# A spectral filter and two expert layers: the last super-tile 498 columns wide, the first loads and products reordered, the last unit ordered for its stores

## The reference

```python
X = np.fft.rfft(x, axis=1)
y = np.fft.irfft(X * (filt_r + 1j * filt_i)[None], n=3008, axis=1)
t = y.reshape(6016, 256)                       # 6016 tokens
h = t @ w_in                                   # layer 1
t = np.where(h > 0, h, np.exp(np.minimum(h, 0)) - 1) @ w_out
h = t @ w2_in                                  # layer 2
out = (h * np.clip(h + 3, 0, 6) / 6) @ w2_out
```

## Time and profile before

| | |
|---|---|
| median of 3 runs | 1104.79 us (1104.62 to 1105.99) |
| the profiled execution's own time | 1103.63 us |
| its span in the trace | 1101.8 us |
| PE busy, DVE, ACT, POOL | 99%, 69%, 70%, 25% |

### The profile page before, as it was taken

The page is one execution under the profiler, slowest core; times in us unless marked ns, Lnnn a source line. Parts: engine busy times, 40 slices in busy tenths (PEclk is TensorE's granted clock), DMA queues, the critical chain, the costliest instruction groups (busy, mean ns, idle before and its releaser), DMA issues.

```text
span 1101.8 us, 13377 instructions
## 1 busy us (share of the span) xinstructions
PE 1093.9 (99%) x4798; PEld 882.8 (80%) x4798; DVE 757.3 (69%) x941; ACT 765.9 (70%) x1149; POOL 280.4 (25%) x215
## 2 busy tenths in 40 slices
PE   9999999999999999999999999999999999999998
PEld 4666878888888888888887888888888888888886
DVE  7998676666666676676687866665665666666665
ACT  0554788788788788888898666566666666666654
POOL 4757051111111111120398620120121021020000
PEclk9999999999999999999999999999999999999999
DMA  9755200200100101101211201001101001000001
GB/s 288 241 173 175 91 1 3 74 1 14 63 1 31 44 1 38 39 1 38 76 58 57 76 1 38 38 1 38 38 1 38 38 1 38 38 1 1 38 1 38
DMA packets 29330, 54.20 MB, mean 49 GB/s; under 512 B 3408, under 2 KB 19664, under 8 KB 29264
## 3 DMA queue, kind: packets, MB, share of 16 engines
q1 hardware_dynamic: 23648, 44.12, 12.0%
q10 hardware_dynamic: 5616, 9.22, 2.5%
HBM read 34.83 MB, written 18.51 MB: 48 GB/s over the span
## 4 chain that ended last, share of the span: by engine, by line
PE 91%; ACT 4%; DVE 2%; issue 1%; POOL 1%; ACTq 0%; POOLq 0%
PE ps L479 43%; PE ps L470 13%; PE ps L468 13%; PE ps L469 13%; PE ps L432 3%; PE ps L400 3%; PE ps L408 2%; DVE e L776 2%; PE ps L417 1%; ACT e L634 1%; ACT w_hi L606 1%; ACT e L636 1%; PE ps L419 1%; PE ps L420 1%; PE ps L438 0%
## 5 line engine op out<-in xcount | busy, mean ns | idle before, releaser
L790 DVE TENSOR_TENSOR g_lo<-e,g_hi 128x502 fp32r<-128x502 f32 (+1 forms) x288 | 276.5, 988 | 135.0 <-ACT g_hi L669 134.3
L468 PE MATMUL ps<-op_hi,w_hi 128*128 128x502 f32 x672 | 261.9, 390 | 0.0
L470 PE MATMUL ps<-op_lo,w_hi 128*128 128x502 f32 x672 | 261.8, 390 | 0.0
L469 PE MATMUL ps<-op_hi,w_lo 128*128 128x502 f32 x672 | 261.2, 389 | 0.0
L479 PE MATMUL ps<-g_lo,w_hi 128*128 128x502 f32 x766 | 236.9, 390 | 1.2 <-DVE g_lo L790 0.9
L479 PE MATMUL ps<-g_hi,w_hi 128*128 128x502 f32 x766 | 235.7, 389 | 0.2 <-ACT g_hi L669 0.2
L479 PE MATMUL ps<-g_hi,w_lo 128*128 128x502 f32 x766 | 234.9, 388 | 0.0
L873 POOL TENSOR_TENSOR op_lo<-op_raw,op_hi 128x1004 fp32r<-128x1004 f32 (+1 forms) x48 | 100.8, 2102 | 448.3 <-ACT op_hi L614 448.1
L479 PEld LDWEIGHTS ps<-g_lo,w_hi 128*128 128x128 f32 x766 | 143.3, 188 | 32.4 <-DVE g_lo L790 3.9
L479 PEld LDWEIGHTS ps<-g_hi,w_hi 128*128 128x128 f32 x766 | 143.7, 188 | 29.9 <-ACT g_hi L669 1.2
L479 PEld LDWEIGHTS ps<-g_hi,w_lo 128*128 128x128 f32 x766 | 144.1, 188 | 29.3
(11 more groups left out here) (74 smaller groups left out, 1147.9 us busy)
## 6 DMA issues: line engine op xcount, KB each, us to landing
op_raw<-y SPq DMA_DIRECT2D x36, 251.0 KB, 3.6
x_ring<-x_dev SPq DMA_DIRECT2D x32, 192.0 KB, 4.9
y<-ystage SPq DMA_DIRECT2D x12, 502.0 KB, 2.9
out_dev<-ystage SPq DMA_DIRECT2D x11, 502.0 KB, 2.9
y<-ystage ACTq DMA_DIRECT2D x18, 235.0 KB, 2.5
f_ring<-f_dev SPq DMA_DIRECT2D x11, 384.0 KB, 6.6
w_raw<-w_dev ACTq DMA_DIRECT2D x16, 256.0 KB, 4.5
w_raw<-w_dev SPq DMA_DIRECT2D x16, 256.0 KB, 3.1
```

Of the source, the lines that this page charges most:

```text
L468: pe.matmul(out, w_hi[p][:, cols], hi, start=start, stop=False, skip_group_check=True)
L469: pe.matmul(out, w_lo[p][:, cols], hi, start=False, stop=False, skip_group_check=True)
L470: pe.matmul(out, w_hi[p][:, cols], lo, start=False, stop=True, skip_group_check=True).then_inc(done, 1)
L790: return dve.tensor_tensor(g_lo[:, tiles, :], e[:, tiles, :], f32(g_hi[:, tiles, :]), ALU.subtract)
```

## The change

Four things change. (1) The last super-tile of each layer has two tiles of `LAST_T` = 498 columns; the padding, its memset and its store go, and the rows of `y0`, `y1` and the output are 6016 long. TensorE's matmuls, GpSimd's sums and the operand splits of that super-tile are 498 wide, ScalarE's and VectorE's work on the activations stays 502 wide. (2) The first `x` tile is loaded from ScalarE's queue ahead of the sign vector, the second takes its place on SyncE's, and the third zero product is 256 columns wide. (3) At `u` = 0 one of the two bank-filling products and the first `up` stand ahead of the wait for group 30. (4) The last unit runs 11, 21, and then 22 and 12 together, first for one output half, then for the other; the last half is stored in two transfers, partitions 0 to 63 from SyncE and 64 to 127 from ScalarE.

```diff
 T = 502
-TOKP = NS * 2 * T
-PAD = TOKP - TOK
+LAST_T = (TOK - (NS - 1) * 2 * T) // 2
...
+        def width(s):
+            return LAST_T if s % NS == NS - 1 else T
...
             sp.dma_start(mat("A"), mats_dev[:, 0:P]).then_inc(mat_loaded["A"], 16)
-            load_x(0)
+            load_x(1)
             sp.dma_start(mat("BX"), mats_dev[:, P:2 * P]).then_inc(mat_loaded["BX"], 16)
-            load_x(1)
             load_x(2)
...
-            sp.wait_ge(zeroed, 2)
-            sp.dma_start(y0[:, :, TOK:].rearrange("o p t -> p o t"), pad_zero[:]).then_inc(pad_stored, 16)
...
-            for o in range(DH):
-                sp.wait_ge(end_evac[o], 1)
-                sp.dma_start(out_dev[o, :, at:at + T], ystage[:, 1, o * T:o * T + T]).then_inc(y_stored[1], 16)
+            sp.wait_ge(end_evac[0], 1)
+            sp.dma_start(out_dev[0, :, at:at + LAST_T], ystage[:, 1, 0:LAST_T]).then_inc(y_stored[1], 16)
+            sp.wait_ge(end_evac[1], 1)
+            sp.dma_start(out_dev[1, 0:P // 2, at:at + LAST_T],
+                         ystage[0:P // 2, 1, T:T + LAST_T]).then_inc(y_stored[1], 16)
...
-            for _ in range(3):
-                pe.matmul(ps[:, 0, :], back[:, 0, 0, :], back[:, 0, 0:4, :].rearrange("p j d -> p (j d)"),
-                          start=True, stop=True)
+            for cols in (4, 4, 2):
+                pe.matmul(ps[:, 0, 0:cols * P], back[:, 0, 0, :],
+                          back[:, 0, 0:cols, :].rearrange("p j d -> p (j d)"), start=True, stop=True)
...
+            def last_columns(n):
+                p = PAIRS - 1
+                pe.wait_ge(lopair, NU)
+                pe.wait_ge(lo12, NU)
+                for o in range(DH):
+                    for fi, tile in ((1, TILE22), (0, TILE12)):
+                        at = (7 + 2 * fi + o) * P
+                        cols = slice(at, at + P)
+                        pe.matmul(out_bank(o, 1)[:, 0:n], w_hi[p][:, cols], g_hi[:, tile, 0:n],
+                                  start=False, stop=False, skip_group_check=True)
...
+                    last.then_inc(last_half if o == 0 else d12_done, 1)
...
-                    pe.wait_ge(back_ready, NG - 1)
-                    for b in (BANK_B, BANK_C):
-                        pe.matmul(bank(b), w_hi[0][:, 0:P], op_hi[0][:, 0, :], start=True, stop=True)
+                    pe.matmul(bank(BANK_B), w_hi[0][:, 0:P], op_hi[0][:, 0, :], start=True, stop=True)
...
                     if u == 0:
+                        pe.wait_ge(back_ready, NG - 1)
+                        pe.matmul(bank(BANK_C), w_hi[0][:, 0:P], op_hi[0][:, 0, :], start=True, stop=True)
                         part_i(LAST_I)
...
+            down(NU - 1, 0, 0, hi11, lo11, True, False, d11_done)
+            down(NU - 1, 1, 0, hipair, lopair, False, True, d21_done)
+            last_columns(LAST_T)
...
+                at = (NS - 1) * 2 * T + LAST_T
+                act.wait_ge(end_evac[1], 1)
+                act.dma_start(out_dev[1, P // 2:P, at:at + LAST_T],
+                              ystage[P // 2:P, 1, T:T + LAST_T]).then_inc(y_stored[1], 16)
...
+            act.dma_start(x_ring[0:AROWS, 0], x_dev[ORDER[0]][:, 0:GCOL]).then_inc(x_loaded[0], 16)
             act.dma_start(sign[:], sign_dev).then_inc(sign_loaded, 16)
```

66 lines of the change are left out of this document (29 added, 37 removed).

## The result

The changed kernel took 1109.84 us (median of 6 runs, 1108.20 to 1111.72) against 1104.73 for the kernel before in the same session: a ratio of 1.0051, 95% interval 1.0041 to 1.0061. Forecast was 1102.0, so even the sign was wrong. The profiled execution took 1110.54, with a span of 1108.7 where the earlier trace rows have 1101.8.

What follows compares the result with a forecast made beforehand. PE (TensorE) was taken to bound the kernel, on the chain for 91% of the span. Gains of 0.4 + 0.2 + 0.74 + 1.4 = 2.74 off the 1104.79 median gave 1102.0 us, range 1101.2 to 1103.3.

Steps and rivals of the forecast that it cites:

- I expect the landing to move as far as PE does: Filter start: group 7's tile, with 0.11 slack, lands as much sooner as PE wants it, 0.4; otherwise 0.3 lost.
- The rival: Filter start: group 7's tile or another keeps its landing, so 0.3 to 0.4 is lost, 1102.4; chance 0.09.
- The clock rival: Start: TensorE's slow pace ends later than 6.95, gain gone at 5.5 later; chance 0.10 including other start trouble.
- The zero product: Start: halving the columns of the third zero product's last two instructions gains 0.41, taken as 0.4.
- The hand-over: Filter to layer 1: products moved into PE's idle time gain 0.2, bounds 0.08 and 0.27, since VectorE is late next.
- The narrower super-tiles: Last super-tile of each layer: four fewer columns save 1.7 ns a matmul, 0.74 in all, bounds 0.6 and 1.2.
- Layer 1's 0.17: Layer 1: only 98 of the 498-wide matmuls lie where PE is the chain, gaining 0.17.
- Layer 1's extra gain: Rival: layer 1's other narrower matmuls also count, 0.45 more, 1101.6; chance 0.08.
- The end: After the last matmul: reordered last unit and lone last store end the span 1.4 sooner, bounds 0.9 and 1.7.
- the split of the last store I price at nothing: Last store: splitting it in two by partitions changes nothing; up to 1.0 more gain if halves ran side by side.
- The rival of a late last store: End: last store lands in 2.5, not 2.0, so the end gains 0.9, time 1102.55; chance 0.18.
- the new place of the `lo12` wait: Last unit: the wait's new place delays the last columns' matmuls, taking 0.05 off the end's gain.

Runs made afterwards that it cites:

- e2: The kernel before with only pad_zero allocated last, so buffers behind its old place move down 64 bytes; 0.49% slower.
- e4: The kernel before with only the change's first loads (first x tile from ScalarE's queue, second in its place on SyncE's); 0.18% slower.
- e1: The changed kernel with an unused 64-byte spacer where pad_zero stood, restoring buffer places; 3.1 us apart from e3.
- f2: f1 with the change's first loads (first x tile from ScalarE's queue, second in its place on SyncE's); 2.2 us over f1.
- f1: The changed kernel with old first loads, first two weight loads one filter step later, spacers moving buffers up, last half in one store; ratio 0.9959 to the kernel before.
- e3: The changed kernel with the 64-byte spacer and the first loads as before the change; 1103.23 us.
- e7: The kernel before with only the change's new end (last unit's order, last half in two stores); end 0.67 us shorter, too little to be timed.
- e9: The kernel before with an unused 64-byte buffer behind op1_lo, so g_hi, g_lo, e and h2 stand 64 bytes higher; 3.6 us over the kernel before.
- e11: e6 with the last output half stored in one transfer from SyncE's queue; end 1.40 us shorter than the kernel before's.
- e6: The changed kernel with the 64-byte spacer, old first loads, and first two layer 1 weight loads one filter step later; 1102.5 us.
- m1: Not the reference kernel: only 128x502 matmuls on zeros, streamed operand shifted by 0 to 224 bytes, other engines idle, then ScalarE and VectorE busy; 10.213 to 10.393 for 45.
- m2: m1 with the operand's slices at pitches of 502, 512, 520 and 528 columns, each at several shifts; 10.050 to 10.394 us for 45 matmuls.

## Why the prediction was wrong

**The sum of what went wrong.** The profiled difference of 6.9 in the span is: 3.1 at the activation of unit 0 (117.47 before, 120.60 now), 4.8 from unit 8 to 88, of which 0.9 is the tie at unit 50, less 0.38 in the last super-tile and 0.75 at the end. The timed 5.1 is less, since the profiled execution had both the tie and the stretch at 1.2 GHz, and only half of the timed ones had the latter. Put together from the single runs it is much the same: in medians the shifted buffers cost 6.1 (e2 over the kernel before) and the loads 2.2 (e4); against e2, whose layout it has, the changed kernel gains 0.5 from unit 8 to 88 and 1.1 from 88 to 95; the zero product, the hand-over and the end give 0.4, 0.3 and 0.7. That leaves 5.3.

**The step that failed first** is one that the prediction doesn't have. It counted what `pad_zero` did (a memset, a store of 8 KB) and took the buffer itself for nothing. Removing it slid `op1_*`, `g_*`, `e` and `h2` by 64 bytes, worth 3.9 us in the units from 8 to 88 alone (822.68 - 817.86 - 0.9). So the step that failed is this term of nothing, with 3.9 in its place. Every term "nothing changes here" rested on that. e2 shows it, e1 undoes it.

**The start's data.** "I expect the landing to move as far as PE does" failed. It took the earlier issue of the first loads for a gain of the whole backlog, and did not ask what stands beside what on two queues. The rival had the mechanism, with 0.3 to 0.4 of loss; measured is 2.2 (e4 over the kernel before, f2 over f1) to 3.1 (e1 over e3). It was mis-sized since only group 7's slack was looked at. Group 5's tile had about a microsecond of it (wanted at 17.2, where the wait of 2.26 begins, landed at 16.43 before), and now landed 2.9 later. The first filter, "covered" and said to go out 0.4 later, landed 2.6 later (7.97 for 5.38).

**The clock rival** was right in kind and wrong in place: the granted clock did fall to the 1.2 GHz level in half of the executions, but at 21 us, behind the stall, not at 7.

**The zero product** was sized right, 0.41, but for a slow pace that ends at a given time. That time is no property of the code. The trace's records of the granted clock begin where the slow pace ends, at 6.93 in the kernel before, 7.35 in the changed one, and from 4.35 (e3) to 7.54 (e7) over the fifteen profiles; the kernel before and e7 have the same start, and differ by 0.6. (Ahead of its first record a view prints 1.00: the prediction's "recorded as full all along" is a reading of no record.) To compare, take two profiles in which the pace ends at nearly the same time. Weight loads get short there, and the first "BX" product follows: e9, with 512 columns,

```profile
7.48 0.19 PEld L401 LDWEIGHTS ps<-x_ring,mats 96*128 96x128 f32 x1 [0.41 <-issue]
...
8.97 0.89 PE L409 MATMUL ps<-spec,mats 128*128 128x384 f32 x2
```

and e11, with 256:

```profile
7.50 0.19 PEld L401 LDWEIGHTS ps<-x_ring,mats 96*128 96x128 f32 x1 [0.43 <-issue]
...
8.56 0.88 PE L409 MATMUL ps<-spec,mats 128*128 128x384 f32 x2
```

That is 0.41. Before the change this product starts at 8.76 and after it at 8.54, only 0.22 earlier, since the slow pace lasted 0.42 longer in that execution and half of this is lost. The means of the six profiles with 512 columns and the nine with 256 are 8.73 and 7.90, twice as far apart, since the slow pace happened to end earlier in the nine, at 5.9 in the mean for 6.9. An estimate by a straight line through all fifteen gives 0.42 for the columns and 0.43 for each microsecond of slow pace.

**The hand-over**: 0.2 forecast. From the last "A" product's start to the activation of unit 0 it took 18.03, and takes 17.77 (102.83 to 120.60), 17.80 in e3, 17.82 in e6: 0.21 to 0.26. Right, and for the reason given: `back` is still waited for, 0.53 at L432.

**The narrower super-tiles**: 0.74 forecast. In the old layout units 88 to 95 take 71.33 before and 71.04 in e3 and e6, so layer 2 gives 0.3 instead of 0.57. A unit of 498 takes 10.13 where one of 502 took 10.19: some 1.3 ns for a matmul, not 1.7, and the first two units of the seven gain next to nothing. Layer 1's 0.17 is not seen: from unit 8 to 88 e1 and e3 take 817.96 and 818.02, the kernel before and e4 817.86 and 817.89. The prediction took the time of a column from 512 and 384 columns and from a mean at 502; it did not know that the time of a matmul depends on the layout as much as on four columns. In the changed kernel's own layout the same edit gave more, 1.12 from unit 88 to 95. Layer 1's extra gain was rightly refused: the two chain pieces around it keep their distance (5.09 and 5.08).

**The end**: 1.4 forecast, 0.75 measured, and 1.40 with one store (e11). The working held for one store: 3.51 against 3.48 behind the last matmul, with the landing at the forecast 2.0, VectorE's evacuation at 1102.13 and well ahead of the last store; only the new place of the `lo12` wait was 0.17 (7.89 from the activation of unit 95 to the last matmul, 7.72 before) where 0.05 was taken. The failed step is "the split of the last store I price at nothing": it costs 0.65. The rival of a late last store (2.5 forecast, 2.7 measured) had two issuing queues as one reason, and was right; the rest of the first half's transfer, its other reason, had nothing to do with it, since e11 has that too and lands at 2.0.

## What to carry to other kernels

Before an edit removes or resizes a buffer, list the addresses of those behind it, and compare the pace of instructions that the edit does not touch; if it moved, restore the layout with a spacer first and judge the edit then. Where loads are a backlog, moving the first of them to another queue reorders all of them: price the landing of every tile, not the one with the least slack. One profile fixes neither the end of the slow pace, worth up to 1.4 us here (7.54 to 4.35, times 0.43), nor a tie between VectorE and GpSimd, worth 0.9: a term below a microsecond needs the same stretch from several executions.

## What the runs showed of the hardware

- The pace of back-to-back matmuls of 128x502 with operands in SBUF depends on the streamed operand's address: 10.213 to 10.393 for 45 in m1, 10.050 to 10.394 in m2, the same to 0.001 with ScalarE and VectorE busy or idle, and again at the same shift.
- In the kernel, 64 bytes of shift are 10.19 against 10.29 a unit, and a shift of other buffers by 128 bytes gives 10.19 for 10.21. At 498 columns a unit takes 10.13 in both layouts.
- Two transfers of 124.5 KB to disjoint partitions from two queues took 0.55 and 0.58 to issue and 2.4 and 2.7 to land, where one of 249 KB took 0.34 and 2.0.
- TensorE's slow pace at the start ended between 4.35 and 7.54 us, with the first zero product at 1.45 in all fifteen profiles.
- A wait of TensorE's weight load of 2.3 us at 17 us was followed by a granted clock of 0.50 from 21 to 24 us, one of 2.5 in e4 by the same from 20.4 to 23.8; in e1, with a wait of 3.0, it stayed at 1.00.
